# A fused attention, mixture-of-experts and feed-forward kernel: the gate made per expert slot, and the zero rows written in eight pieces

## The reference

```python
# attention: packs gather from k and v, then the queries gather from the packs
p_packed = sm_attn(p, k, v)
out = sm_attn(q, p_packed, p_packed)
x = out.transpose(0, 2, 1, 3).reshape(4608, 512)
# mixture of experts: each token goes to its best expert, scaled by its gate
logits = x @ w_gate
expert_idx = np.argmax(logits, axis=1)
probs = np.exp(logits - logits.max(-1, keepdims=True))
probs /= probs.sum(-1, keepdims=True) + 1e-09
gate_w = probs[np.arange(N), expert_idx]
out[mask] = gate_w[mask, None] * (np.maximum(xe @ w1[e], 0.0) @ w2[e])
# dense
g = s * np.maximum(x @ w_in, 0.0) ** 2 + b
return g @ w_out
```

## Time and profile before

| | |
|---|---|
| median of 3 runs | 1559.7 us (1558.63 to 1560.64) |
| the profiled execution | 1560.72 us, of which the span of the profile is 1559.0 us |
| mean granted clock of PE | 0.969 |
| PE, PE weight loads | 94%, 76% of the span |
| DVE, ACT, POOL | 30%, 31%, 27% of the span |
| bytes moved by DMA | 122.78 MB, mean 79 GB/s |

### The profile page before, as it was taken

One profiled execution on the slowest core, in us unless ns is written; L12 is line 12 of the kernel. 1 busy time (PEld: TensorE's weight loads), 2 busy tenths in 40 slices (PEclk: granted clock), 3 DMA queues, 4 the chain that ended last, 5 costly groups with the idle time before them and its releaser, 6 DMA issues.

```text
span 1559.0 us, 24694 instructions
## 1 busy us (share of the span) xinstructions
PE 1468.7 (94%) x8664; PEld 1181.3 (76%) x8665; DVE 474.2 (30%) x808; ACT 480.7 (31%) x973; POOL 416.0 (27%) x278
## 2 busy tenths in 40 slices
PE   6888559999999999998999999999999999999996
PEld 5555448888888888886888888888888888888885
DVE  3666731111111111113523233332323233332322
ACT  5555323333333333332222222222222222222221
POOL 0344469356274565203601010100101010010100
PEclk9898669999999999999999999999999999999998
DMA  9778344233242343213201010000101000000000
GB/s 308 220 244 254 107 139 162 94 122 110 85 148 86 116 135 104 91 34 102 68 14 37 12 40 13 34 13 13 40 7 41 13 34 13 13 27 0 27 1 27
DMA packets 52850, 122.78 MB, mean 79 GB/s; under 512 B 6608, under 2 KB 12752, under 8 KB 52816
## 3 DMA queue, kind: packets, MB, share of 16 engines
q1 hardware_dynamic: 33728, 79.21, 16.3%
q10 hardware_dynamic: 13136, 24.19, 5.0%
q0 software_dynamic: 5952, 18.92, 3.5%
HBM read 90.78 MB, written 31.52 MB: 78 GB/s over the span
## 4 chain that ended last, share of the span: by engine, by line
PE 90%; DVE 3%; issue 2%; DMA 1%; ACT 1%; POOL 1%; another core or an unknown queue 0%; SPq 0%; ACTq 0%; DVEq 0%; POOLq 0%
PE psum L657 18%; PE psum L659 18%; PE psum L658 18%; PE psum L733 8%; PE psum L732 8%; PE psum L731 8%; PE psum L701 2%; PE psum L490 2%; PE psum L666 1%; PE psum L719 1%; PE psum L551 1%; PE psum L530 1%; PE psum L592 1%; DMA q_sb<-in_q_dram 1%; PE psum L605 1%
## 5 line engine op out<-in xcount | busy, mean ns | idle before, releaser
L1224 DVE SCALAR_TENSOR_TENSOR s_r_r<-r_relu,s_col 128x512 f32<-128x512 f32 x144 | 116.2, 807 | 449.5 <-ACT r_relu L955 449.5
L465 POOL DMA_INDIRECT out_dram<-out_sb,out_row_of_y x36 | 35.6, 990 | 746.9 <-ACT out_sb L965 738.6
L657 PE MATMUL psum<-weights_split,gT_hi 128*128 128x512 f32 x576 | 230.9, 401 | 2.4 <-DVE gT_lo L1226 2.3
L955 ACT ACTIVATE r_relu<-psum 128x512 f32<-128x512 f32 x144 | 86.1, 598 | 470.9 <-PE psum L733 453.7
L658 PE MATMUL psum<-weights_split,gT_hi 128*128 128x512 f32 x576 | 227.7, 395 | 0.0
L659 PE MATMUL psum<-weights_split,gT_lo 128*128 128x512 f32 x576 | 227.7, 395 | 0.0
L733 PE MATMUL psum<-yT_hi,weights_split 128*128 128x512 f32 x576 | 227.2, 394 | 0.0
L731 PE MATMUL psum<-yT_hi,weights_split 128*128 128x512 f32 x576 | 225.7, 392 | 0.0
L732 PE MATMUL psum<-yT_lo,weights_split 128*128 128x512 f32 x576 | 225.5, 391 | 0.0
L396 POOL TENSOR_TENSOR weights_split<-weights_raw,one 128x1024 fp32r<-128x1024 f32 x70 | 135.3, 1933 | 254.5 <-PE psum L659 244.5
L398 POOL TENSOR_TENSOR weights_split<-weights_raw,weights_split 128x1024 fp32r<-128x1024 f32 x70 | 169.7, 2424 | 5.5
(11 more groups left out here) (151 smaller groups left out, 1850.6 us busy)
## 6 DMA issues: line engine op xcount, KB each, us to landing
weights_raw<-in_moe_w_dram SPq DMA_DIRECT2D x64, 512.0 KB
x_slot<-x_by_expert ACTq DMA_DIRECT2D x40, 257.0 KB, 2.7
y_sorted<-y_slot ACTq DMA_DIRECT2D x40, 256.5 KB, 3.0
k_sb<-in_k_dram SPq DMA_DIRECT2D x16, 576.0 KB
q_sb<-in_q_dram SPq DMA_DIRECT2D x16, 576.0 KB, 7.4
v_sb<-in_v_dram SPq DMA_DIRECT2D x48, 192.0 KB
y_tile<-y_sorted SPq DMA_DIRECT2D x32, 256.5 KB, 2.6
weights_raw<-in_moe_w_in_dram SPq DMA_DIRECT2D x8, 512.0 KB
```

The source lines that it names most:

```text
L657: nc.tensor.matmul(dst, lhs[0][:, col:col + P], rhs[0], start=first_, stop=False)
L955: nc.scalar.activation(rel[:], ps[:, HFB + par, :], ACT.Relu).then_inc(rel_done, 1)
L1224: nc.vector.scalar_tensor_tensor(sq[par][:], rel[:], s_col[:], rel[:], ALU.mult, ALU.mult).then_inc(sq_done, 1)
```

## The change

A row of x is now 521 floats: 512 of x, eight logits, and the token's number. No gate is made in the attention stage: `shifted`, `exp_logits` and `gates` are gone, and POOL's last addition of the logits writes straight into the x row. In the expert stage, DVE takes the negated maximum of the eight logits of a slot (`max_slot`), ACT makes the exponential with its sum (`exp_slot`) and DVE adds 1e-09 and takes the reciprocal (`gate_slot`). Gate and token number go into one column per slot of two tables, in place of the three small tiles.

The zero rows are written by eight DMAs of 128 rows, two in each of the steps 4 to 7 on ACT's queue. For this, POOL's order changes: `scatter(0)` stands behind `sum_logits(1)` and waits for all eight. The token numbers of the first four batches are copied at once, at the start of POOL's stream.

```diff
-XW = DM + 2
+XW = DM + E + 1
@@ POOL
-                nc.gpsimd.tensor_tensor(lg[:, b * J:(b + 1) * J, :]..., lg2[:, 0, :], lg2[:, 1, :], ALU.add).then_inc(lg_done, 1)
+                need(pool, x_sent[b % XBUFS], BATCH_DMA * (b // XBUFS))
+                nc.gpsimd.tensor_tensor(x_rows[:, b % XBUFS, :, DM:DM + E], lg2[:, 0, :]..., lg2[:, 1, :]..., ALU.add).then_inc(lg_done, 1)
...
+            pool.wait_ge(id_steps, 3)
+            pool.wait_ge(pt_full, 4)
+            nc.gpsimd.tensor_copy(x_rows[:, :, :, DM + E], ids[:, 0:XBUFS, :]).then_inc(ids_done, 1)
             round_low(0)
-            pool.wait_ge(zeroed, 16)
-            pool.wait_ge(id_steps, 3)
             for b in range(B):
-                if b >= 1:
+                if b >= 2:
                     scatter(b - 1, 0)
                 sum_logits(b)
+                if b == 1:
+                    pool.wait_ge(ids_done, 2)
+                    pool.wait_ge(zeroed, 16 * E)
+                    scatter(0, 0)
                 if b >= 1:
                     scatter(b - 1, J // 2)
                 if b + 1 < EARLY:
@@ ACT, attention
-            act.wait_ge(zeros_done, 1)
-            act.dma_start(rows_dram.rearrange("(e r) c -> r e c", e=E)[0:P],
-                          zeros[:].unsqueeze(1).to_broadcast([P, E, XW])).then_inc(zeroed, 16)
             for it in range(UNITS + 1):
                 if it < UNITS:
                     out_q(it)
-                if it >= 5 and it % 2 == 1:
-                    exp_logits((it - 5) // 2)
+                if it == 4:
+                    act.wait_ge(zeros_done, 1)
+                if 4 <= it < 8:
+                    for e in (2 * it - 8, 2 * it - 7):
+                        act.dma_start(rows_dram[e * REG:e * REG + P, :], zeros[:]).then_inc(zeroed, 16)
@@ ACT, experts
-                nc.scalar.copy(ysb[:, DM:], gid[age][:, 1:2])
-                nc.scalar.activation(ysb[:, 0:DM], ps[:, YB, :], ACT.Copy, scale=gid[age][:, 0:1]).then_inc(y_done, 1)
+                act.wait_ge(sgate_done, s + 1)
+                nc.scalar.activation(ysb[:, 0:DM], ps[:, YB, :], ACT.Copy, scale=slot_gate[:, bass.ds(s, 1)])
+                nc.scalar.copy(ysb[:, DM:], slot_id[:, bass.ds(s, 1)]).then_inc(y_done, 1)
...
-            def keep_columns(s, n):
...
+            def exp_slot(s):
+                act.wait_ge(smax_done, s + 1)
+                need(act, seps_done, s)
+                nc.scalar.activation(slot_exp[:], xin[:, DM:DM + E], ACT.Exp, bias=slot_max[:], accum_out=slot_sum[:]).then_inc(sexp_done, 1)
+                nc.scalar.copy(slot_id[:, bass.ds(s, 1)], xin[:, DM + E:]).then_inc(sid_done, 1)
+                act.wait_ge(sexp_done, s + 1)
+                act.wait_ge(sid_done, s + 1)
@@ DVE
-                need(dve, exp_out, b)
-                nc.vector.tensor_tensor(shifted[:], lgb, mx[:]..., ALU.subtract).then_inc(exp_in, 1)
...
-            def gates(b):
...
             def positions(b):
-                gates(b)
...
+            def max_slot(s):
+                dve.wait_ge(xin_in, 16 * s + 16)
+                need(dve, sexp_done, s)
+                nc.vector.tensor_reduce(slot_max[:], xin[:, DM:DM + E], AX.X, ALU.max, negate=True).then_inc(smax_done, 1)
+
+            def gate_slot(s):
+                dve.wait_ge(sexp_done, s + 1)
+                nc.vector.tensor_scalar_add(slot_sum_eps[:], slot_sum[:], EPS).then_inc(seps_done, 1)
+                dve.wait_ge(seps_done, s + 1)
+                nc.vector.reciprocal(slot_gate[:, bass.ds(s, 1)], slot_sum_eps[:]).then_inc(sgate_done, 1)
...
             with dve.Fori(1, before3 + 2) as s:
+                max_slot(s + 1)
                 x_lo(s + 1)
+                gate_slot(s + 1)
                 h_lo(s)
```

More of the change, by code:

```diff
@@ L144, in build @@
         out_row = sb("out_row_of_y", [P, TOK], I32)
-        gid = [sb(f"gate_and_token{i}", [P, 2]) for i in range(3)]
+        slot_gate = sb("gate_of_slot_row", [P, SLOTS])
+        slot_id = sb("token_of_slot_row", [P, SLOTS])
+        slot_max = sb("slot_minus_max", [P, 1])
+        slot_exp = sb("slot_exp", [P, E])
+        slot_sum = sb("slot_sum_of_exp", [P, 1])
+        slot_sum_eps = sb("slot_sum_eps", [P, 1])
         y_at = sb("slot_y_row", [1, SLOTS], I32)
@@ L407, in sum_logits @@
                 pool.wait_ge(lgt, 2 * b + 2)
-                nc.gpsimd.tensor_tensor(lg[:, b * J:(b + 1) * J, :].rearrange("p j e -> p (j e)"), lg2[:, 0, :], lg2[:, 1, :],
-                                        ALU.add).then_inc(lg_done, 1)
+                need(pool, x_sent[b % XBUFS], BATCH_DMA * (b // XBUFS))
+                nc.gpsimd.tensor_tensor(x_rows[:, b % XBUFS, :, DM:DM + E], lg2[:, 0, :].rearrange("p (j e) -> p j e", j=J),
+                                        lg2[:, 1, :].rearrange("p (j e) -> p j e", j=J), ALU.add).then_inc(lg_done, 1)
             def scatter(b, j0):
                 pool.wait_ge(pos_done, b + 1)
[L414 to L417, removed]
+                if j0 == 0 and b >= XBUFS:
+                    pool.wait_ge(x_sent[b % XBUFS], BATCH_DMA * (b // XBUFS))
+                    nc.gpsimd.tensor_copy(x_rows[:, b % XBUFS, :, DM + E], ids[:, b, :]).then_inc(ids_done, 1)
+                    pool.wait_ge(ids_done, b + 3 - XBUFS)
                 for j in range(j0, j0 + J // 2):
@@ L828, in round_high @@
                 nc.scalar.copy(part(n // NCH * WBUF, 0, n % NCH * CH, CH), raw[n % 2][:]).then_inc(hi_done, 1)
-            def exp_logits(b):
-                act.wait_ge(exp_in, b + 1)
-                nc.scalar.activation(powers[:], shifted[:], ACT.Exp).then_inc(exp_out, 1)
             for g in (0, 2):
@@ L919, in _ @@
             x_hi(0)
-            keep_columns(0, 0)
+            exp_slot(0)
             load(1)
@@ L923, in _ @@
             x_hi(1)
-            keep_columns(1, 1)
+            exp_slot(1)
             load(2)
@@ L929, in _ @@
                 x_hi(s + 1)
-                keep_columns(s + 1, 2)
+                exp_slot(s + 1)
                 load(s + 2)
-                y_out_(s - 1, 2)
+                y_out_(s - 1)
                 h_hi(s)
@@ L935, in _ @@
             x_hi(before3 + 2)
-            keep_columns(before3 + 2, 2)
-            y_out_(before3, 2)
+            exp_slot(before3 + 2)
+            y_out_(before3)
             for t in range(GT):
@@ L983, in _ @@
                 y_hi(0, i, yT[0], i % 2)
-            y_out_(before3 + 1, 1)
+            y_out_(before3 + 1)
             for i in range(2, GT):
@@ L987, in _ @@
             h_hi(before3 + 2)
-            y_out_(before3 + 2, 0)
+            y_out_(before3 + 2)
             block_(0, 0)
@@ L1020, in experts @@
             def experts(b):
-                lgb = lg[:, b * J:(b + 1) * J, :]
+                lgb = x_rows[:, b % XBUFS, :, DM:DM + E]
                 em8_ = em8[:].unsqueeze(1).to_broadcast([SP_, J, E])
@@ L1027, in experts @@
                 dve.wait_ge(dr, 4 * b + 1)
-                need(dve, exp_out, b)
-                nc.vector.tensor_tensor(shifted[:], lgb, mx[:].unsqueeze(2).to_broadcast([SP_, J, E]), ALU.subtract).then_inc(exp_in, 1)
                 nc.vector.tensor_tensor(eq[:], lgb, mx[:].unsqueeze(2).to_broadcast([SP_, J, E]), ALU.is_equal).then_inc(dr, 1)
```

31 lines of the change are left out of this document (9 added, 22 removed).

## The result

The changed kernel takes 1570.43 us (median of 5 runs, 1567.85 to 1571.6), the kernel before on the same chip 1560.64 (1558.63 to 1562.02): ratio 1.005 with a 95% interval of 1.0034 to 1.0066, slower. The profiled executions, 1570.65 and 1560.72 us, have spans of 1568.6 and 1559.0, so the traces have 9.6 us to explain.

| up to | before, us | after, us | moved by |
|---|---|---|---|
| start of step 3 (`score_keys`) | 40.02 | 36.81 | -3.2 |
| start of step 6 | 70.29 | 69.55 | -0.7 |
| start of step 8 | 91.25 | 85.56 | -5.7 |
| start of step 9 | 101.45 | 106.05 | +4.6 |
| start of step 15 | 164.84 | 168.01 | +3.2 |

A forecast was written before the change was run, and what follows sets the result against it. PE was taken to bound the expert stage, DMA the start, and a DVE, ACT and PE path the attention steps. Terms -5.0 + 0.3 + 4.1 - 1.5 = -2.1 us gave 1558.6, median 1557.6, range 1553 to 1562.

The forecast's parts named there:

- The span from the first slot on unchanged: Sign that the forecast is right: the expert stage and all behind it take as long as before, cost 0.
- The cover for the gate per slot: Expert stage: new ACT and DVE work hides beside busy PE, ACT waiting 4.51 us per slot; cost 0.
- The stall of step 8: Attention stage: DVE waits for POOL, held by the last zero piece; 3.6 us stall, +4.1 us with clock effects.
- Z + 15.0 - 97.40: Step 8: DVE's stall is last landing plus 15.0 us of POOL's queue, less `experts(2)`'s old start; 3.6 us.
- Z: Time the last zero piece lands, taken as 86.0 us, between 83.2 and 87.9.
- rival C: Step 8: wait for the last piece outweighs the gains from a landing at 88 us on; up to 1570, chance 0.09.
- The rule on turns between queues: DMA engines alternate queues by packet; equal turns would land the last piece near 85 us, sum 1 us lower; not adopted.
- The start: Step 2: without the zero DMA PE's k and q waits go and the clock stays up; -5.0 us.
- near 35: Sign that the forecast is right: step 3 starts near 35 us, with no DMA wait of PE in step 2.
- The pieces: Steps 4 to 7: two zero DMA issues per step on ACT pass nearly hidden; +0.3 us (0 to +1.5).
- `shifted` and `gates`: Attention stage: removing these DVE operations saves 3.1 us, half given back to pauses; -1.5 us (-3.1 to 0).
- rival E: Expert stage: ACT loads a table in every slot, +3 to +5 us on the sum, 1561.6; chance 0.05.

The follow-up runs named there:

- b_pad: Kernel before with 32 unused bytes ahead of the tiles of the expert and dense stages: 1550.48 us, ratio 1.0052.
- b_pad128: Kernel before with 128 unused bytes ahead of the tiles of the expert and dense stages: 1530.87 us, ratio 0.9954.
- b_zero8: Kernel before with only the eight zero DMAs in steps 4 to 7 and POOL's new order: 1551.41 us, ratio 1.007.
- b_pad64: Kernel before with 64 unused bytes ahead of the tiles of the expert and dense stages: 1541.72 us, ratio 1.0022.
- a_best160: Changed kernel with one zero DMA ahead of step 0, POOL's old order and 160 unused bytes: 1531.67 us, ratio 0.9807 to the kernel before.
- a_order: Changed kernel with 96 unused bytes and POOL's sum_logits(2) ahead of the wait for the pieces: 1531.52 us, ratio 0.9949 to the kernel before.
- a_early: Changed kernel with 96 unused bytes and the eight pieces issued in steps 3 to 5: 1532.84 us, ratio 0.9955 to the kernel before.
- second batch: Four versions of the changed kernel with 96 unused bytes, varying pieces and POOL's order, on a chip where the kernel before took 1539.89 us.
- a_best: Changed kernel with one zero DMA ahead of step 0, POOL's old order and 96 unused bytes: 1531.04 us, ratio 0.9942 to the kernel before.
- first four batches: Follow-up runs on other chips, testing the change's parts, the wait and tile addresses against the kernel before; that kernel took 1541.71, 1539.89, 1539.21 and 1534.75 us.
- b_pad192: Kernel before with 192 unused bytes ahead of the tiles of the expert and dense stages: 1516.87 us, one run.
- b_pad192r: Kernel before with 192 unused bytes ahead of the expert and dense tiles, timed again in five runs: 1537.43 us, ratio 0.9839.
- fifth batch: Two kernels at equal tile positions, with and without the gate per slot, on a chip where the kernel before took 1561.74 us.

## Why the prediction was wrong

Forecast 1557.6 us (1553 to 1562), measured 1570.43. Two steps failed. The first by itself puts the time outside the range. The second, by itself, would too, but other terms of the attention stage gave part of it back: as a whole that stage missed its forecast by 4.2 us.

**"The span from the first slot on unchanged"** failed: it grew by 7.5 us. Of these 5.3 are the dense stage's pace, which the prediction had put at nothing because nothing in that stage was touched; b_pad shows that 32 bytes between two tiles do it, and b_pad128 that they can do the reverse. The other 2.3 lie where the two stages meet, and are within what executions differ by there: from the fortieth slot load to the first result rows the 20 traces take 139.3 to 145.3 us, 140.8 before and 143.0 after among them, and 144.8 in b_zero8, whose tiles lie as before. The cover for the gate per slot held: no gap of PE, 4.85 us of idle time on ACT, 12.53 against 12.52 us a slot.

The Trainium skill ("SBUF — State Buffer", Operand start alignment) asks that an operand start at a multiple of its element size, and says that this is about legality and not speed. Both kernels keep it; the runs show 2.8% between two addresses that do (91.41 and 88.94 us).

**The stall of step 8** was named, but sized 4.1 us; step 8 grew by 10.3. The step that failed is `Z + 15.0 - 97.40`. DVE was due at 85.56 + (97.40 - 91.25) = 91.7 and started at 100.96, so it waited 9.3 us, not 3.6. Three things make the 5.7 between:

- The last piece took 7.9 us from issue to landing, not 5.5: 2.4.
- From the landing to `experts(2)` POOL took 100.96 - 85.5 = 15.5 us, not 15.0: 0.5.
- Both ends of the wait moved, and not by the same: the last issue came 2.9 us earlier than forecast (77.57, not 80.5), the need 5.7 earlier (91.7, not 97.40). Step 7 lies between the two, and it took 7.8 us in place of 10.9: 2.8.

The third is what I hadn't seen at all: steps 6 and 7 lost their scatters, and 5.0 us with them. The gain at the start, which lies ahead of both ends, doesn't change the wait; the gain of step 7 only made it longer. That Z itself was right, 86.0 forecast and 85.5 measured, is luck: the issue was 2.9 us early and the landing 2.4 us longer. On the forecast's own time scale Z was 80.5 + 7.9 = 88.4, just past the 88 from which rival C counted; to that comes a need that came earlier, which C hadn't either.

The rule on turns between queues ("DMA: Bandwidth & Descriptors" in the Trainium skill, Queues, rings and completion order), with equal turns, would have had Z near 85, which is 4.5 us from the issue that the forecast assumes; the trace has 7.9 us, so it doesn't bear out equal turns.

**The start.** The waits went as told and step 3 began at 36.81 ("near 35"). The gain is 3.2 us, not 5.0: in this execution the clock fell in step 1 instead. That can't be put down to the change, as step 1 takes 9.5 to 9.7 us in b_pad128, b_pad64 and a_best160 too, which have the zero DMA ahead of step 0, and 7.2 in a_order, a_early and b_zero8, which don't. The term was also read from one execution. Over all traces step 3 starts at 39.05 us on average with the zero DMA ahead of step 0 (14 traces, 37.27 to 41.77) and at 36.35 without (6, 34.98 to 38.19): 2.7 us. In a_best160 no turn in step 2 waits even with the zero DMA there.

**The pieces.** +0.3 was forecast "nearly hidden", steps 4 and 5 grew by 2.5 us, and in the second batch by 2.9. The two issues were sized at 0.4 us each from the one in the trace; the first pair took 2.09, ahead of the copy that PE waits for, the later ones 0.82 to 0.84. What makes step 5 longer wasn't tried.

**`shifted` and `gates`.** -1.5 was forecast; 2 to 6 us are measured. The half that I gave back for the pauses of `mix_packs` was not given back: most odd steps fell from 8.2 or 8.3 us (b_pad128) to 7.8 to 8.0 (a_best).

**Table loads** (rival E): one, as forecast from the earlier trace rows, which agrees with the Trainium skill ("ScalarE: Activation LUTs", Table sets), where relu and copy are in every set.

In terms: start -3.2 (-5.0), pieces +2.5 (+0.3), steps 6 and 7 -5.0 (not forecast), step 8 +10.3 (+4.1), steps 9 to 14 and the way to the first slot -2.5 (-1.5) make +2.1 at the first slot (-2.1); expert stage +2.3 and dense stage +5.3 (0 and 0).

## What to carry to other kernels

The price of a wait is its release less the moment its result is needed, and a change can move both. A gain ahead of both leaves the price as it is; a gain between what starts the release and the need is eaten by the wait. Ask of each wait what stands behind it in its queue: the same operations in another order were worth 9 to 11 us here. And when a change alters the size of any tile, list the start addresses of all tiles behind it before comparing times, because 32 bytes moved this kernel by 0.5% and 192 by 1.6%.

## What the hardware showed that I had not expected

**Addresses.** With PE busy without a gap, the mean 128 x 512 product of a line takes 389 to 401 ns by the positions of its operands in SBUF within 256 bytes, the stationary one's included, though the weight loads have 187 to 189 ns at all of them. Of the five positions tried, 128 was best in both stages. weights_split, the other operand, starts at byte 16512, which is 128 past a multiple of 256 as well; whether it is the equal position that helps, or 128 by itself, wasn't tried.

**Chips.** The kernel before took 1534.75 to 1541.71 us in the first four batches, and 1559.7 to 1561.74 us beside the changed kernel and in the fifth. The difference lies in the attention stage, in the steps with scatters: the first slot is loaded at 189.27 us in b_pad192 and at 208.51 in b_pad192r, the same kernel. PE's `mix_packs` in step 9, with three scatters, in the second batch (a_best), and in the fifth (a_best160, the same code but for 64 unused bytes):

```profile
97.71 1.25 PE L600 MATMUL psum<-pkx,a2T 32*96 32x73 f32 x48
```

```profile
103.55 0.90 PE L600 MATMUL psum<-pkx,a2T 32*96 32x73 f32 x29 [0.65 <-DVE a L1064]
104.63 0.22 PE L600 MATMUL psum<-pkx,a2T 32*96 32x73 f32 x1 [0.18 <-issue]
105.34 0.72 PE L600 MATMUL psum<-pkx,a2T 32*96 32x73 f32 x18 [0.49 <-issue]
```

In the fifth batch such pauses stand in the stretches in which POOL issues indirect DMAs and just behind them, and most steps from 6 on take 9.9 to 11.2 us (10.1 in a_best160) in place of 7.8 to 8.3. Without scatters (steps 6 and 7 of the changed kernel) it takes 7.8 to 8.2 on such a chip too, which fits the 5.0 us that these steps lost; that it is the scatters was not tried by itself. Why one chip does it and another doesn't stays open.
